# A fused attention, mixture-of-experts and token-mixing kernel: the value product turned round, gate logits taken in attention, expert slots gathered instead of scattered

## The reference

```python
# attention, for each of 4 batches and 8 heads
s = q @ k.T / 8
s = where(s >= s.max(-1) - tau, s, -1e9)
p = exp(s - s.max(-1))
x = (p / (p.sum(-1) + 1e-9)) @ v          # heads side by side: (4, 576, 512)

# experts, token after token of a batch
logits = x @ w_gate                       # 8 experts
fresh = argmax(logits)
e = fresh if first or sigmoid(x @ w_local) < 0.5 else e_of_the_token_before
x = softmax(logits)[e] * (relu(x @ w1[e]) @ w2[e])

# mixing
theta = x @ w_theta
y = w_tok_r @ (x * cos(theta)) + w_tok_i @ (x * sin(theta))
out = (x + y) + relu((x + y) @ w_ch)
```

## Time and profile before

| | us |
|---|---|
| median of three runs (lowest, highest) | 957.26 (953.88, 958.52) |
| the profiled execution | 956.66 |
| its span, first to last instruction | 954.8 |
| PE busy (share of the span) | 854.5 (89%) |
| PEld busy | 729.1 (76%) |
| DVE busy | 504.7 (53%) |
| ACT busy | 419.4 (44%) |
| POOL busy | 479.7 (50%) |

### The profile page before, as it was taken

One profiled execution on the slowest core, in us unless ns is written; L12 is line 12 of the kernel. 1 busy time (PEld: TensorE's weight loads), 2 busy tenths in 40 slices (PEclk: granted clock), 3 DMA queues, 4 the chain that ended last, 5 costly groups with the idle time before them and its releaser, 6 DMA issues. The chain is left out here.

```text
span 954.8 us, 18680 instructions
## 1 busy us (share of the span) xinstructions
PE 854.5 (89%) x6093; PEld 729.1 (76%) x6094; DVE 504.7 (53%) x1051; ACT 419.4 (44%) x727; POOL 479.7 (50%) x423
## 2 busy tenths in 40 slices
PE   2989999999999654899999999999475999999998
PEld 2878888888888432788888888888354999898998
DVE  4989999999998460122212221221374664655722
ACT  2677777777777522122211222122354543434300
POOL 2565655756663034925798779930267341513200
PEclk9999999999999955899999999999786999999999
DMA  8565676577569015633455455641210011110001
GB/s 218 128 180 159 167 187 184 154 179 204 139 152 312 2 63 183 209 108 110 147 193 169 161 166 182 205 163 44 92 47 28 23 43 36 45 56 1 32 20 50
DMA packets 69941, 117.90 MB, mean 123 GB/s; under 512 B 28049, under 2 KB 32401, under 8 KB 69905
## 3 DMA queue, kind: packets, MB, share of 16 engines
q1 hardware_dynamic: 59904, 95.13, 34.0%
q10 hardware_dynamic: 7056, 12.85, 4.1%
q0 software_dynamic: 2944, 9.44, 3.0%
HBM read 64.70 MB, written 24.38 MB: 93 GB/s over the span
## 5 line engine op out<-in xcount | busy, mean ns | idle before, releaser
L202 POOL TENSOR_SCALAR p_ring<-p_ring,rsum 128x576 f32<-128x576 f32 x144 | 105.9, 745 | 122.7 <-DVE rsum L271 122.7
L345 PE MATMUL psum<-k_st,q_st 128*128 128x288 f32 x640 | 126.3, 326 | 29.4 <-DMA q_st<-q_split 15.7
L781 POOL TENSOR_TENSOR w_lo<-w_raw,w_hi 128x1024 fp32r<-128x1024 f32 x56 | 134.5, 2401 | 4.7
L345 PEld LDWEIGHTS psum<-k_st,q_st 128*128 128x128 f32 x640 | 94.7, 198 | 45.1 <-issue 31.3
L239 DVE TENSOR_REDUCE negmax<-psum 128x1 f32<-128x576 f32 x144 | 107.7, 748 | 30.3 <-PE psum L345 30.2
L421 ACT COPY p_t<-psum 128x512 f32<-128x512 f32 (+1 forms) x224 | 111.9, 499 | 23.6 <-PE psum L358 18.9
L251 DVE SCALAR_TENSOR_TENSOR p_ring<-psum,thresh,e_ring 128x576 f32<-128x576 f32 x144 | 116.6, 810 | 0.7 <-ACT e_ring L397 0.5
L397 ACT ACTIVATE e_ring<-psum,negmax 128x576 f32<-128x576 f32 x144 | 107.2, 744 | 21.1 <-DVE negmax L239 19.5
L1174 PE MATMUL psum<-tok_hi,z_hi 128*128 128x288 f32 x288 | 87.5, 304 | 11.2 <-DVE z_lo L1077 11.2
L369 PE MATMUL psum<-p_t,v_sb 128*64 128x128 f32 (+1 forms) x1600 | 96.8, 267 | 0.4 <-ACT p_t L421 0.4
L358 PE MATMUL psum<-ident,p_ring 128*128 128x128 f32 x576 | 89.7, 278 | 1.9 <-ACT p_t L421 1.8
(11 more groups left out here) (177 smaller groups left out, 1786.8 us busy)
## 6 DMA issues: line engine op xcount, KB each, us to landing
w_raw<-w_dram SPq DMA_DIRECT2D x60, 512.0 KB, 3.5
k_st<-k_split SPq DMA_DIRECT2D x64, 288.0 KB, 4.9
q_st<-q_split SPq DMA_DIRECT2D x64, 144.0 KB, 2.5
xs_dram<-zeros SPq DMA_DIRECT2D x14, 512.0 KB, 3.2
xs_nat<-xs_dram ACTq DMA_DIRECT2D x26, 256.0 KB, 2.7
ys_dram<-y_nat ACTq DMA_DIRECT2D x23, 256.0 KB, 2.1
k_nat<-k_t_dram SPq DMA_DIRECT2D x16, 288.0 KB, 4.3
q_nat<-q_t_dram SPq DMA_DIRECT2D x16, 288.0 KB, 4.6
```

Source lines behind the costliest of these rows:

```text
L202: pl.tensor_scalar(t, t, rsum[:, k % BODY:k % BODY + 1], 1.0, ALU.mult, ALU.mult).then_inc(s_norm, 1)
L345: mm = pe.matmul(bank[:, x, 0:HALF], lhs, key[:, HALF * x:HALF * x + HALF], start=(j == 0), stop=(j == len(terms) - 1))
L781: lo = pl.tensor_tensor(w_lo[:, m % 2, r // 4, part], raw[:, r % 4, :], w_hi[:, m % 2, r // 4, part].bitcast(F32), ALU.subtract)
```

## The change

Six things are changed.

1. *Value product.* The transposed probabilities become the stationary operand (128 keys x 128 queries), and V moves, with 74 columns: 64 of V, nine of V times the gate weights, and a column of ones (L504 of the new kernel). The result is token rows: x, its share of the gate logits, and the sum of the probabilities. A new group "g" computes the nine columns once per pair, with five matmuls of `v_nat` and `gates` (L489). The group order gains "g" ahead of the first "t".
2. *Sums and division.* The mask has no accumulation, and `sum_eps`, `recip` of the tiles and GpSimd's `norm` are gone. The results go to `x_tmp`, two of the five blocks through VectorE (`take`) and three through ScalarE. Twice per pair GpSimd adds 1e-9 to the sums, VectorE takes the reciprocal, and GpSimd multiplies x (`x_fin`) and the logits (`lg`) with it (`finish`).
3. *Leads.* Scores run three tiles ahead of the groups instead of seven, exponentials two instead of six, and masks none instead of five; `p_ring` has six tiles. `row_thresh` reads -tau from PSUM.
4. *x goes to DRAM.* SP stores each pair's `x_fin` to `x_dram` (`store_x`). The parts of `xs_dram` are no longer cleared. The first q halves are stacked by ScalarE's queue.
5. *Weights.* Expert 0's weights are loaded and split within attention, on GpSimd (`split_piece`: two pieces in the round before the last, six in the last), expert 1's in the routing, also on GpSimd, and the rest in the expert stage.
6. *Routing and gathering.* The logits are one sum over `lg`. x is not transposed any more and there is no scatter. Behind `index` new steps turn "row of each token" into "token of each row" (`source`): tile and place within the tile (`digit`), `put` (token number where the tile matches, 500 elements) and `hot_lane` (one-hot of the place, five times 512), and twenty fp32 matmuls that add them up. GpSimd gathers two slots at the end of the routing into `xs_nat`, and the other 23 at the start of the expert stage, from where SP stores them to `xs_dram` for ScalarE's loads.

The diff, cut to what the steps below speak of (`load_piece` and the new semaphores are as described):

```diff
+def split_piece(pl, w, feed, e, r):
+    part = slice((r % 4) * PIECE, (r % 4 + 1) * PIECE)
+    raw = feed["raw"][:, r % 4, :]
+    hi, lo = (w[n][:, (e + 1) % 2, r // 4, part] for n in ("hi", "lo"))
+    pl.wait_ge(feed["raw_in"][r % 4], 32 * e + 16 * (r // 4) + 16)
+    pl.tensor_scalar(hi, raw, 1.0, 1.0, ALU.mult, ALU.mult).then_inc(feed["whi"], 1)
+    pl.wait_ge(feed["whi"], PIECES * e + r + 1)
+    pl.tensor_tensor(lo, raw, hi.bitcast(F32), ALU.subtract).then_inc(feed["raw_free"], 1)
...
-    GROUPS = TILES + FULL + 1 + FULL + 1
-    AHEAD_S, AHEAD_E, AHEAD_M = 7, 6, 5
...
+    AHEAD_S, AHEAD_E = 3, 2
...
+    def step_groups(u):
+        c = u // 2
+        if u == 0:
+            return [("g", 0), ("t", u)]
+        if u == TILES - 1:
+            return [("t", u), ("pv", 3), ("k", 4), ("pv", 4)]
+        if u % 2:
+            return [("t", u), ("k", c)]
+        return [("t", u), ("pv", c - 1)]
...
+    DVE_C = (1, 3)
...
+        def store_x(b, hp, m):
+            cols = slice(hp * P, hp * P + P)
+            rows = d["x"].rearrange("(b s) n -> b s n", b=BATCH)[bass.ds(b, 1), :, cols]
+            sp.dma_start(rows[:, 0:FULL * P, :].rearrange("o (t p) n -> p (o t) n", p=P),
+                         x_fin[m][:, 0:FULL, :]).then_inc(s_xst[m], 16)
...
-        def norm(i, k):
-            hold(s_rsum, BATCHES * i + k // BATCH_OF + 1)
-            t = p_ring[:, k % RING, :]
-            pl.tensor_scalar(t, t, rsum[:, k % BODY:k % BODY + 1], 1.0, ALU.mult, ALU.mult).then_inc(s_norm, 1)
...
+        def finish(i, m, late):
...
+            hold(s_free_act, 2 * N_ACT * i + N_ACT * m + ACT_DONE[last + 1])
+            hold(s_free_dve, 2 * N_DVE * i + N_DVE * m + DVE_DONE[last + 1])
+            pl.tensor_scalar(rs[m][:, cs, :], x_tmp[m][:, cs, :, W - 1], 1e-9, 1.0, ALU.add, ALU.mult).then_inc(s_eps, 1)
+            hold(s_rs, 4 * i + 2 * m + late + 1)
+            if not late:
+                hold(s_xst[m], 32 * i + 32)
+            factor = rs[m][:, cs, :].unsqueeze(3)
+            pl.tensor_tensor(x_fin[m][:, cs, :].rearrange("p c (h e) -> p c h e", h=2), x_tmp[m][:, cs, :, 0:D],
+                             factor.to_broadcast([P, n, 2, D]), ALU.mult).then_inc(s_fin, 1)
+            pl.tensor_tensor(lg[:, cs, bass.ds(2 * i + m, 1), :].rearrange("p c o (h e) -> p (c o) h e", h=2),
+                             x_tmp[m][:, cs, :, D:D + G], factor.to_broadcast([P, n, 2, G]), ALU.mult).then_inc(s_fin, 1)
...
+                for _ in range(pieces[m]):
+                    split_piece(pl, w, feed, 0, at + pieces[2])
+                    at += 1
+                finish(i, m, 0)
+                finish(i, m, 1)
...
+        with pl.Fori(0, ITER - 2) as i:
+            body(i, True, (0, 0, 0))
+        body(ITER - 2, True, (1, 1, 0))
+        body(ITER - 1, False, (4, 2, 2))
...
         def row_thresh(i, k):
...
+            n = BODY * i + k
+            first = isinstance(i, int) and n == 0
+            if not first:
+                dve.wait_ge(s_exp, n)
+            dve.wait_ge(s_max, n + 1)
             dve.scalar_tensor_tensor(out=thresh[:, k % 3:k % 3 + 1], in0=negmax[:, k % 3:k % 3 + 1], scalar=-1.0,
-                                     in1=neg_tau[:], op0=ALU.mult, op1=ALU.add).then_inc(s_thr, 1)
+                                     in1=neg_tau[:] if first else s_bank[(k - 1) % 3][:, 0, CONST:CONST + 1],
+                                     op0=ALU.mult, op1=ALU.add).then_inc(s_thr, 1)
...
-                in1=e_ring[:, k % 2, :].rearrange("p (a b) -> p a b", a=2), op0=ALU.is_ge, op1=ALU.mult,
-                accum_out=sums[:, k % BODY:k % BODY + 1]).then_inc(s_mask, 1)
...
-                dve.tensor_scalar(rsum[:, cols], sums[:, cols], 1e-9, None, ALU.add).then_inc(s_sum, 1)
...
+        def take(i, m, c):
+            q = PV_AT[c]
+            dve.wait_ge(s_fin, 8 * i + 4 * m + FIN_START - 4)
+            dve.wait_ge(s_filled, 2 * GROUPS * i + GROUPS * m + q + 1)
+            dve.tensor_copy(x_tmp[m][:, c, :, :], misc[q % 2][:, 0:2 * W].rearrange("p (h e) -> p h e", h=2)
+                            ).then_inc(s_free_dve, 1)
...
+            dve.wait_ge(s_eps, 4 * i + 2 * m + late + 1)
+            dve.reciprocal(rs[m][:, cs, :], rs[m][:, cs, :]).then_inc(s_rs, 1)
...
+            if what == "g":
...
+                for t in range(KT):
+                    at = t * P if t < FULL else S - P
+                    rhs = gates[:, bass.ds(2 * i + m, 1), :].rearrange("p o n -> p (o n)")
+                    mm = pe.matmul(bank[:, t * 2 * G:(t + 1) * 2 * G], v_nat[m % 2][:, at:at + P], rhs,
+                                   start=True, stop=True)
+            elif what == "t":
...
             else:
...
-                n = REM if arg == 4 else P
-                for t in range(KT):
-                    for h in range(2):
-                        mm = pe.matmul(bank[D * h:D * h + D, 0:n], v_sb[m][:, h, t, :], p_t[arg % 2][:, h, t, 0:n],
+                    pe.wait_ge(s_v[m % 2], 64 * i + 64 * (m // 2) + 64)
+                for h in range(2):
+                    for t in range(KT):
+                        mm = pe.matmul(bank[:, h * W:(h + 1) * W], p_t[arg % 2][:, h, t, :], v_sb[m % 2][:, h, t, :],
                                        start=(t == 0), stop=(t == KT - 1))
...
-                dst = xT[:, bass.ds(2 * i + m, 1), P * arg:P * arg + n].rearrange("p o q -> p (o q)")
-                src = bank[:, 0:n]
-            act.copy(dst, src).then_inc(s_free, 1)
+                act.wait_ge(s_fin, 8 * i + 4 * m + FIN_START - 4)
+                dst = x_tmp[m % 2][0:n, arg, :, :]
+                src = bank[0:n, 0:2 * W].rearrange("p (h e) -> p h e", h=2)
...
+        act.wait_ge(s_qlo, 1)
+        for h, at in ((0, 0), (1, S + REM)):
+            for t in range(2):
+                act.dma_start(q_st[0][t * D:t * D + D, at:at + S].bitcast(F32),
...
-        def w_low(r):
...
+        link(v.memset(where[:], 0.0))
+        link(v.tensor_reduce(logits[:], lg[:].rearrange("p t (b c) (h e) -> p (t b) e (c h)", b=BATCH, h=2), AX.X, ALU.add))
...
         link(v.tensor_copy(keep["index"][0:n, 4, :], where[0:n, 4, :]), "index")
...
+        tile, place = digit[:, 0, :], digit[:, 1, :]
+        link(v.tensor_scalar(tile, flat, 1.0 / P, -127.0 / 256.0, ALU.mult, ALU.add))
...
+        link(v.scalar_tensor_tensor(out=place, in0=tile, scalar=-float(P), in1=flat, op0=ALU.mult, op1=ALU.add))
+        link(v.tensor_tensor(put[:], C["slot_ids"][:, 0:SLOTS].unsqueeze(1).to_broadcast([P, TT, SLOTS]),
+                             tile.unsqueeze(2).to_broadcast([P, TT, SLOTS]), ALU.is_equal))
+        link(v.tensor_tensor(put[:], put[:], C["token"].unsqueeze(2).to_broadcast([P, TT, SLOTS]), ALU.mult))
+        for t in range(ST):
+            link(v.tensor_tensor(hot_lane[t], C["lane"].unsqueeze(1).to_broadcast([P, BATCH, P]),
+                                 place[:, BATCH * t:BATCH * t + BATCH].unsqueeze(2).to_broadcast([P, BATCH, P]),
+                                 ALU.is_equal), f"hot{t}")
+        v.wait_ge(s_lane, 5)
+        link(v.tensor_copy(keep["source"][:], psum[:, 2, 0:SLOTS]), "source")
...
-        def to_rows(j):
...
-            for c in range(DC):
-                mm = pe.transpose(psum[0:n, 1 + j % 2, c * P:c * P + P], xT[:, b * DC + c, t * P:t * P + n], ident[:])
...
-            to_rows(j)
+        for t in range(ST):
+            n = TOKENS[t]
+            pe.wait_ge(step, STEP[f"hot{t}"])
+            for b in range(BATCH):
+                mm = pe.matmul(psum[:, 2, 0:SLOTS], hot_lane[t][0:n, b, :], put[0:n, BATCH * t + b, :],
+                               start=(t == 0 and b == 0), stop=(t == ST - 1 and b == BATCH - 1))
+        mm.then_inc(s_lane, 1)
...
-        for r in range(PIECES):
-            dst = slice((r % 4) * PIECE, (r % 4 + 1) * PIECE)
-            act.copy(w["hi"][:, 0, r // 4, dst], w["raw"][:, r, :]).then_inc(s_whi, 1)
...
-        for j, (b, t) in enumerate(tiles):
...
-            act.copy(x_nat[0:n, j % NX, :], psum[0:n, 1 + j % 2, :]).then_inc(s_nat, 1)
...
-        pl.wait_ge(step, STEP["index"])
-        for j, (b, t) in enumerate(tiles):
-            n = TOKENS[t]
-            pl.wait_ge(s_nat, j + 1)
-            pl.indirect_dma_start(out=d["xs"], out_offset=bass.IndirectOffsetOnAxis(ap=keep["index"][0:n, t, b:b + 1], axis=0),
-                                  in_=x_nat[0:n, j % NX, :], in_offset=None).then_inc(s_scatter[j % NX], 16)
...
+        for r in range(PIECES):
+            split_piece(pl, w, feed, 1, r)
+        for m in range(2):
+            pl.wait_ge(s_xst[m], 32 + 32 * BATCH * DC // 2)
+        pl.wait_ge(step, STEP["source"])
+        for j in range(2):
+            pl.indirect_dma_start(out=xs[:, j, :], out_offset=None, in_=d["x"],
+                                  in_offset=bass.IndirectOffsetOnAxis(ap=keep["source"][:, j:j + 1], axis=0)
+                                  ).then_inc(s_first[j], 16)
...
+        for j in range(2, SLOTS):
...
```

(26 more changed lines are left out.)

518 lines of the change are left out of this document (264 added, 254 removed).

## The result

The changed kernel takes 1037.76 us (median of 4 runs, 1035.81 to 1038.59), the kernel before 956.37 (4 runs, 953.88 to 958.52): 1.085 times as long, 95% interval 1.082 to 1.088. The profiled execution took 1037.80 us with a span of 1036.1. Forecast were 1024 us and a range of 990 to 1055.

What follows compares the result with a forecast made beforehand. In attention TensorE and VectorE were near full, and TensorE was to become the later engine. Terms: 956.66 - 1 + 80 - 5.5 + 2.5 - 9 = 1024 us (start, loop, fill, tail, routing); range 990 to 1055.

Steps and rivals of the forecast that it cites:

- The loop, +80 us: Attention's 16 pairs: 23.4 us each instead of 18.39, set by loads of fp32 stationary tiles; +61 to +106.
- rival 1: Attention's value product: loading fp32 weights does not set the pace, pair 18.3 us, whole kernel 943 us; chance 10%.
- VectorE and ScalarE hidden: Attention's loop: VectorE stays near 15 us per pair, ScalarE keeps 18 of 19 copies; both hidden behind TensorE.
- The fill, -5.5 us: Start of attention's pipeline: three score tiles ahead instead of seven, 5.8 us in place of 11.3.
- The start, -1 us: Before attention: q tiles issued on ScalarE's queue beside SP's k tiles; -1 us (-2 to 0).
- The tail, +2.5: End of attention: copy, add, reciprocal, product and x's store behind the last value group add 2.5 us.
- Routing, -9 us: Routing stage: the experts' first transpose at 50 us, with VectorE slowed by GpSimd's splitting; -9 us (-20 to -1).
- Experts and mixing, 0: Expert and mixing stages: no change in time; a few us lost once if the cover for slot 2 is short.
- the second: Attention's value and gate products: load and streaming in turn, pair 30 us, +186, whole kernel 1130 us; chance 4%.
- The third: TensorE's granted clock falls within attention; a quarter of the loop at half speed costs 94 us, 1118 us; chance 4%.

Runs made afterwards that it cites:

- cols37: Changed kernel with the value product moving only 37 of its 74 columns, the other columns of x left out; 1055.07 us (one run).
- gate_twice: Changed kernel with each of the five gate matmuls per pair issued twice, same result; 1058.58 us (one run).
- no_side: Kernel before, with both heads' value products on the array's left half, so not side by side; 1020.18 us (one run), only attention read.
- split_later: Changed kernel with expert 1's weights split by GpSimd in the expert stage, behind the 23 gathers, instead of in the routing; 1024.35 us (4 runs).
- gather_only: Kernel before with only the change's gathering, expert 0's weights split in the routing as before; 947.29 us (4 runs), 0.991 times before.
- best: Kernel before with the gathering, threshold and sum through PSUM, and the reciprocal ahead of the mask; 936.39 us (5 runs), 0.980 times before.

## Why the prediction was right, and where it was off

1. *The loop, +80 us: right, and for the reason given.* 23.36 us per pair against 23.4, 16 x 4.97 = +79.5. The load-bound record is 0.108 us (0.109 foreseen), the gates 1.08 (1.1), the load 192 ns. One support of that price does not hold, though: the loads of `row_pos` that follow at 0.11 us are transposes at the low level (0.50), at which a record of an fp32 product with 128 stationary columns takes 0.217 us (L791). Such a transpose thus costs half of what an fp32 record does, and if it scales with the clock as the record does, it spoke for rival 1's 0.054 us. The price rested on the other rows alone. `cols37` shows that streaming is not the bound, `gate_twice` that each further full load costs 0.109, `no_side` that what is lost is two 64-column tiles at work at once, worth 4.0 of the 5.0 us.
2. *VectorE and ScalarE hidden: right.* 15.4 us per pair against "near 15".
3. *The fill, -5.5 us: off by 1.9.* Attention grew by 75.9 = 79.5 - 3.6. In the changed kernel TensorE still transposes at the low level at 27.75 us. In `split_later`, whose attention is the same code, four score matmuls take 0.77 us at 21.88 us, where the changed kernel's take 1.30 at 21.97: the clock had risen by then. Its first value group began at 26.44 instead of 29.22, and its attention ended 2.7 us earlier. This term varies from kernel to kernel by more than its error.
4. *The start, -1 us: wrong sign.* The first product came at 17.09 instead of 15.68. The q halves were issued earlier (7.79 against 9.15 us), but landed after a median of 6.4 us instead of 3.4: the DMA engines are busy for 87% or more of every microsecond from 7 us on (81% or more before, until 15 us). The gates and `v_nat` are new there, and the identity now comes behind the stacked k, beside the q halves. I had priced the issue and not the transfer. No run tested this.
5. *The tail, +2.5: right.* From the last matmul to the routing's first VectorE operation it went from 0.8 (321.1 to 321.9) to 3.4 us.
6. *Routing, -9 us: the term that was mis-sized.* From its start to the first transpose it is 57.9 us instead of 58.7: -0.8, outside the -20 to -1 that the prediction gave this term and the 35 to 57 us that it gave the stage. The mechanism held (`source` at 49.2 us; I had weighed 31.5 and 52 and taken 46), and `split_later` shows it by taking it away: 33.0. `source` itself came 3.2 us later than taken. The larger part of the miss is what follows it: 8.8 us against 4. The first gather started 3.2 us after `source` (454.19 - 450.98), where I had taken 0.3 from the scatters; the first transpose comes behind both gathers, where I had counted one. The 3.2 us are seen in the three kernels in which GpSimd splits in the routing (3.1 to 3.3), and 0.9 to 1.0 us in the three in which it does not (`split_later`, `gather_only`, `best`); why GpSimd is slower to start there stays open.
7. *Experts and mixing, 0: right* (+0.5 and +1.6 of 574 us).

Of the rivals, the first (load not the bound, 943 us) is refuted by `cols37`; the second (load and streaming in turn, 1130) by the same run, since the streaming could go without a trace. So the sentence of the Trainium skill (TensorE: Matmul & The Clock Gate, The mechanism, under "What overlaps and what doesn't") by which a load overlaps a running matmul only in another row group does not describe these full tiles. The third did not happen in the changed kernel, but it is near: `cols37` has it in nine of fourteen pairs (0.87 and 0.93 in those shown), and `gate_twice`, with 74 moving columns and twenty gate records, has 0.93 in three. The 4% went by the 1.00 of the loop before, where TensorE was busy for 96% of the time; in these two runs it was busier and its clock fell. In the routing, a comparison of two SBUF operands ended with GpSimd's instruction (2.40 us instead of 0.33), while in attention the maximum, which reads PSUM, kept its length (752 ns, 747 before). The Trainium skill's rule (SBUF — State Buffer, Who interferes with whom) says so, and the trace agrees.

The sum was 1023.7, given as 1024, and the result 1037.8: +1.4 - (-1) = 2.4 us from the start, 1.5 from loop, fill and tail, 8.2 from the routing and 2.1 from experts and mixing, together 14.2, against 14.1 measured. Nearly all of these errors have the same sign, so the total was not saved by cancelling; the loop, which is nearly all of the change, was right within 0.5 us.

## What to carry to other kernels

Count an fp32 product with a small moving operand by its loads: at full clock two records of 0.108 us for 128 stationary columns, whether 18, 37 or 74 columns move. Two 64-column tiles side by side halve the cost of a record, and a turned product gives that up. Relieving an engine that was busy for 92% of a loop brought nothing here, because it did not set the length: see first who waits for whom. And work put on GpSimd beside a chain of small VectorE operations is paid by the chain, here 16 us for eight pieces; moving them to the expert stage cost 5.4 us there and made the whole 13.4 us shorter.
